# The weights' buffer of an expert's slot: chosen by a register in the products' addresses instead of by a branch between two copies of the code

## What is computed

```python
def _moe2_ref(x, w_gate, w_output_gate, w1, w2):
    logits = x @ w_gate                    # x: 2304 x 512
    e_idx = np.argmax(logits, axis=1)      # one of 8 experts for each token
    ...
    for e in range(E):
        mask = e_idx == e
        h = np.maximum(x[mask] @ w1[e], 0.0)   # 512 -> 1024
        ye = h @ w2[e]                         # 1024 -> 512
        out[mask] = gate_w[mask, None] * eom[mask, e, None] * ye
```

## Time and profile before

| what | us |
|---|---|
| median of three runs | 857.03 |
| the profiled execution, its own time | 863.49 |
| its span, first to last instruction | 861.7 |
| PE busy | 827.6 (96%) |
| VectorE busy | 572.5 (66%) |
| ScalarE busy | 383.6 (45%) |
| GpSimd busy | 180.2 (21%) |
| slots 3 to 26, first product to the last row of products | 636.3 to 851.3 |

### The profile page before, as it was taken

How to read it: one execution, slowest core, us unless ns; L and a number is a source line. 1 busy time by engine, 2 the same in 40 slices (tenths; PEclk the granted TensorE clock), 3 DMA queues, 4 the chain that set the end, 5 groups by cost and what they waited for, 6 DMA issues and landing times.

```text
span 861.7 us, 19310 instructions
## 1 busy us (share of the span) xinstructions
PE 827.6 (96%) x7018; PEld 549.2 (64%) x7019; DVE 572.5 (66%) x1200; ACT 383.6 (45%) x798; POOL 180.2 (21%) x208
## 2 busy tenths in 40 slices
PE   7999999999999999999999999999899999999995
PEld 5888777876555555555455555556577767777773
DVE  4778788877887998998898898855532444222221
ACT  5766667776555555555555555523111111111110
POOL 4444376663000001001001001010121222111100
PEclk9999999999999999999999999999999999999998
DMA  7255565541483884875784875485253852656610
GB/s 223 98 178 180 166 205 181 177 136 61 172 286 132 267 257 173 267 258 172 256 256 183 256 256 183 162 300 193 92 182 139 313 197 76 238 201 219 233 70 14
DMA packets 76554, 163.83 MB, mean 190 GB/s; under 512 B 39574, under 2 KB 43926, under 8 KB 69840
## 3 DMA queue, kind: packets, MB, share of 16 engines
q1 hardware_dynamic: 70576, 146.20, 50.3%
q0 software_dynamic: 5760, 16.80, 5.7%
q10 hardware_dynamic: 160, 0.07, 0.0%
HBM read 109.44 MB, written 47.47 MB: 182 GB/s over the span
## 4 chain that ended last, share of the span: by engine, by line
PE 70%; DVE 12%; issue 6%; DMA 5%; ACT 3%; POOL 2%; another core or an unknown queue 1%; DVEq 0%; POOLq 0%; ACTq 0%; SPq 0%
PE ps L876 18%; PE ps L865 15%; PE ps L971 11%; PE ps L959 11%; DMA arena<-split 4%; PE ps L781 4%; PE ps L726 3%; PE ps L753 3%; ACT arena L1073 2%; DVE arena L1256 2%; DVE arena L1510 2%; POOL arena L555 1%; PE ps L740 1%; DVE yrow L1475 1%; DVE relu L1566 1%
## 5 line engine op out<-in xcount | busy, mean ns | idle before, releaser
L865 PE MATMUL ps<-arena,w_in_sb 128*128 128x384 f16 x1152 | 200.9, 326 | 0.0
L876 PE MATMUL ps<-w_out_sb,arena 128*128 128x512 f16 x576 | 171.2, 379 | 5.0 <-DVE stage L1571 4.9
L865 PEld LDWEIGHTS ps<-arena,w_in_sb 128*128 128x128 f16 x1152 | 112.3, 98 | 80.9
L959 PE MATMUL ps<-x_sb,arena 128*128 128x128 f16 x2112 | 121.7, 219 | 3.9 <-DMA arena<-split 3.0
L959 PEld LDWEIGHTS ps<-x_sb,arena 128*128 128x128 f16 x2112 | 119.3, 98 | 8.1 <-issue 4.9
L1233 ACT ACTIVATE x_sb<-ps 128x512 f16<-128x512 f32 x54 | 31.6, 596 | 206.7 <-PE ps L959 172.4
L971 PE MATMUL ps<-arena,x_sb 128*128 128x512 f16 x528 | 119.7, 383 | 2.2 <-DVE x_sb L1667 2.2
L876 PE MATMUL ps<-w_out_sb,stage 128*128 128x512 f16 x288 | 109.1, 379 | 0.0
L1073 ACT ACTIVATE arena<-ps,arena 128x128 f32<-128x128 f32 x288 | 79.4, 382 | 55.4 <-DVE arena L1258 51.2
L1205 ACT ACTIVATE arena<-relu 128x384 f16<-128x384 f32 x96 | 50.0, 521 | 109.5 <-DVE relu L1566 108.3
L876 PEld LDWEIGHTS ps<-w_out_sb,arena 128*128 128x128 f16 x576 | 55.8, 98 | 65.4 <-issue 7.2
(11 more groups left out here) (210 smaller groups left out, 976.9 us busy)
## 6 DMA issues: line engine op xcount, KB each, us to landing
arena<-split SPq DMA_DIRECT2D x36, 1024.0 KB
arena<-in_moe_w SPq DMA_DIRECT2D x16, 2048.0 KB
split<-arena SPq DMA_DIRECT2D x16, 2048.0 KB, 7.5
arena<-in_qkt SPq DMA_DIRECT2D x15, 576.0 KB, 6.2
stage<-in_moe_w_in SPq DMA_DIRECT2D x16, 512.0 KB, 4.1
stage<-in_moe_w_out SPq DMA_DIRECT2D x16, 512.0 KB, 5.3
x_sb<-rows POOLq DMA_DIRECT2D x27, 257.0 KB
arena<-in_v SPq DMA_DIRECT2D x32, 128.0 KB, 4.4
```

The source lines that it names most:

```text
L865: last = nc.tensor.matmul(ps[:, HB[f % GB], 0:BN], w_in_sb[:, lw, c, f * P:(f + 1) * P], xt[:, a, lx, c, :], start=c == 0 and lw + lx == 0 ...
L876: last = nc.tensor.matmul(ps[:, YB + r, :], g_sb[lg_][:, f % GB, r * P:(r + 1) * P], w_out_sb[:, lw, f, :], start=f == 0 and lg_ + lw == 0 ...
L959: last = nc.tensor.matmul(ps[:, bank, f % 4 * P:(f % 4 + 1) * P], w1_sb[b][:, lw, c, f * P:(f + 1) * P], xgt[:, a, lx, c, :], start=c == 0 ...
```

## The change

Both copies of a used slot become one. The buffer `b` is no number of the code any more but the register `parity`, and the address of each piece of weights is worked out from it on the chip. The early slots still pass a number, and keep their fixed addresses.

```diff
+            def w1_of(b, lw, c, f):
+                if isinstance(b, int):
+                    return w1_sb[b][:, lw, c, f * P:(f + 1) * P]
+                return whole[:, bass.ds(b * (4 * UW) + ((lw * DC + c) * EF + f * P), P)]
+
+            def w2_of(b, lw, f):
+                if isinstance(b, int):
+                    return w2_sb[b][:, lw, f, :]
+                return whole[:, bass.ds(b * (4 * UW) + (2 * UW + (lw * EFC + f) * DM), DM)]
...
-                                                    w1_sb[b][:, lw, c, f * P:(f + 1) * P], xgt[:, a, lx, c, :],
+                                                    w1_of(b, lw, c, f), xgt[:, a, lx, c, :],
...
-                        last = nc.tensor.matmul(ps[:, 6 + a, :], hg[:, a, lh, f, :], w2_sb[b][:, lw, f, :],
+                        last = nc.tensor.matmul(ps[:, 6 + a, :], hg[:, a, lh, f, :], w2_of(b, lw, f),
...
-                    with pe.If(parity):
-                        used_slot(s, a, turn, more, need, 1)
-                    with pe.Else():
-                        used_slot(s, a, turn, more, need, 0)
+                    used_slot(s, a, turn, more, need, parity)
```

## The result

The change made the kernel slower. The median of four runs is 898.75 us (898.57 to 899.37) against 858.53 us for the kernel before beside it: a ratio of 1.0464, with a 95% interval of 1.0425 to 1.0503. That is 40.2 us more; 914 were forecast, with 873 to 973 as range. The profiled execution of after took 898.68 us, and its span is 896.9 us. In the lines of after L969 is L959 of before, L981 is L971, L978 is L968 and L1038 is L1028.

What follows compares the result with a forecast made beforehand. The array bounds the kernel before; the sequencer would bound the changed stage, with a period of 13.8 us, 15.9 with an empty slot. The stage's 57.4 us over the 857.0 median gave 914.4, rounded to 914; range 873 to 973.

Steps and rivals of the forecast that it cites:

- The bound: In the experts' stage the array sets the pace now; after the change PE's sequencer would, 0.281 us against 0.168 per three products.
- The groups: 80 added groups of register operations a slot, 64 in first products and 16 in second, each costing PE's sequencer 0.10 us.
- Loads and products: In the first products, each register-addressed weight load costs the sequencer 0.022 us and each product 0.005 us.
- The rest of the period: Sequencer work per slot beside 9.0 us of first products, giving a period of 13.8 us, 15.9 with an empty slot.
- The half of the second products: Half of a slot's second products costs the sequencer 4 x 0.281 = 1.12 us before the next slot.
- the way into the next slot: From leaving the block to the next slot's products: 1.8 us in the mean, 3.9 with an empty slot between.
- The sum of 57.4: Stage loss in us: 2.8 for the first used slot, then 3.7, 19.5 and 31.4 for two, five and eleven intervals.
- lower case: Engine instructions with register addresses cost the sequencer 0.005 us: period 12.0 us, loss 23 us, time 880 us.
- A: Not slower: a group costs only its record, about 0.05 us, three products 0.13, hidden under the array; 855 to 857; chance 0.08.
- B: Much slower: a register-addressed load costs PE's sequencer 0.05 to 0.10 us, giving 973 to 1076 us; chance 0.10 above 0.05.
- C: A gain: without the second copy, jumps over it are short; at most 1.6 us saved, 855 us; chance 0.02.
- What would show it: Signs in PE's profile: rows of 96 about 9 us, gaps put down to the sequencer, period 13 to 15 us, second products unchanged.

Runs made afterwards that it cites:

- two addresses: The change with only two register addresses, 2 groups in place of 64, for a slot's 96 first products: 857.84 us, ratio 1.0009 to the kernel before.
- The runs with smaller copies: Two runs against the kernel before: only second products by register, 864.53 us (1.0083); only their second half, the branch choosing copies of the rest, 863.26 us (1.0027).
- the first products alone: The change with only first products by register, second products in two copies behind a branch: 892.07 us, ratio 1.0403; with fixed-address second products and no branch, 893.55 us.
- the last run: Against the kernel before, only the second half of the second products by register, the branch choosing copies of the rest: 863.26 us, ratio 1.0027.

## Why the prediction was right, and where its terms were off

**The bound.** Right: the array set the pace before, and the sequencer does now. 64 groups take 8.2 us against 5.4 us of the array, and with the groups taken away (two addresses) the time is that of before.

**The groups.** The term was 0.100 us each, after four register instructions in a row. It is 0.124, and 0.128 with every eighth: a record of 0.046 and 0.078 beside it where engine instructions stand between two groups, against some 0.05 to 0.06 between register instructions alone. By this term the forecast was too low, 64 x 0.028 = 1.8 us a slot.

**Loads and products.** The terms were 0.022 for a load with an address from a register, after VectorE, and 0.005 for a product, after 24 instructions in 0.1 us: 0.081 for three. They are nothing that can be measured: groups with two and with four engine instructions between them keep the same pitch, and 96 register-addressed loads without groups run at the array's pace. By this step the forecast was too high, 32 x 0.081 = 2.6 us a slot. This is the step that failed: the room of half of 0.2 us was read as a price for each instruction, and VectorE's remainder as a price for its address. On PE no such price shows beside a pitch that is paid once for each register instruction; what VectorE's remainder is stays open. And the 0.2 us was no price in the first place: in finer digits the branch of L1031 starts at 738.327, 0.02 us after the array starts the seventh second product, and until then 35 instructions are handed on and not started, in 17 of the 19 slots alike. That is the limit that the experiments found, already at work in the kernel before. The two errors together leave 0.281 for three products against 0.256, 9.0 us for 96 against 8.2; that they nearly cancel is luck.

**The rest of the period.** The half of the second products was 1.12 and is 1.02 (8 groups, 779.96 to 780.98); the wait for the hidden values 1.5, and the second wait's record starts 1.6 us behind the end of the first products' groups; the way into the next slot 1.8, and is 2.0 and 1.6 in turn. With the measured 8.2 and 1.02 put in, the same sum is 8.2 + 1.5 + 0.1 + 1.02 + 1.8 + 0.1 + 0.15 = 12.87 us, against 12.83 in the trace. The forecast had 13.8, and 15.9 for 14.68 with an empty slot. The sum of 57.4 becomes 38.9: the eleven intervals 21.3 for 31.4, the five 12.9 for 19.5, the two 2.6 for 3.7, the single slot 2.2 for 2.8. Its lower case, 880 with engine instructions at 0.005, came with the group at 0.100 and is about as far off on the other side (19 us below, 914 is 15 above).

**The rivals.** A (not slower) fails because a group costs more than its record. Its deciding point, 0.202 us for three products, holds as far as it was tried: at 0.192 plain slots are at 11.05 us, and most of the loss lies where empty slots stand, as A's sum had it (5 us; 6.4 measured in all). B (a dear load) falls with the run of two addresses. The 62 ns that the Trainium skill has for a matmul whose decode is in microcode (page "TensorE: Matmul & The Clock Gate", section "Wait — 56ns, not 53.3ns?") would have given 997 by the prediction's estimate; no run here shows them, and with two addresses 96 register-addressed products start 0.056 us apart. C (a gain from the jumps) is right about its 1.6 us and finds no net time: in the run with two addresses the second products' groups lose as much behind empty slots, and in the change the first products' groups cost far more. The runs with smaller copies show that what a jump costs depends on how much work the array has queued ahead of it; moving it to a worse place was more than half of a loss of 7 us.

**What would show it.** Rows of about 9 us were expected, with gaps put down to the sequencer. The rows are 7.1 to 8.3 us, and there are no gaps: overlapping records hide them, so the place to look is the length of a row and the pitch of the groups. The period of 12.83 us lies just under the 13 to 15 that were named. The second products stayed at 5.3, the clock at 1.00, and the stage begins no later than it did (632.6 us, 636.3 before).

**What the sum left out.** A limit on how far the sequencer may run ahead. In the change it does not bind: the sequencer is 1.0 to 1.4 us ahead at the start of a slot, up to 11 groups, at the edge of the 35 instructions. With a shorter path it would have, and so the same sum fails for the first products alone: 21 us by it, 35 measured.

## What to carry to other kernels

Where an address comes from a register, count the register instructions that the build puts between the engine's instructions (the order shows them), and compare their pitch with the engine time between them: here 0.128 us against 0.084 us of array for each address, while the same groups between products of 0.22 us cost a plain slot nothing. A branch that is taken once for a whole block is cheap as long as the engine has enough work queued to cover its jump, so put it behind long instructions, and keep small, dense ones at fixed addresses. And do not trust an engine's busy share when its records overlap: compare how long the same row of instructions takes.

## What the runs showed of the hardware that was not expected

A group of register operations on PE costs its record and 0.078 us, as long as engine instructions stand between (0.046 to 0.124, 0.092 to 0.170, 0.153 to 0.232), and it makes no difference whether these are 2 or 4, or have an address from a register. Even the 16 of eight transposes fit in: L945's group starts at 778.249 with a record of 0.042, and the next register instruction at 778.369. Every eighth group or so is 0.03 us later.

The sequencer of PE hands on up to 35 engine instructions that the array has not started, and then waits. So a lead is worth 17 products, which is 1 us of first products and 3.7 us of second ones.

The first jump past another copy of the code held the sequencer for 3.0 us in the kernel before, 3.75 us in the last run, and 4.7 us where it stalled three instructions behind the jump. The Trainium skill says ("Runtime: NRT & Kernel Launch", section "Instruction fetch mechanics") that a taken branch to code outside the fetched window waits for its transfer. The trace agrees: each of the three stalls holds one packet of 16 KB in the DMA queue for instructions. The rows of the DMA view over the three stalls, in the same order (queue, packets, MB, share of 16 engines):

```profile
q8 instruction: 1, 0.02, 1.9%
...
q8 instruction: 1, 0.02, 1.5%
...
q8 instruction: 1, 0.02, 1.2%
```

In finer digits the sequencer goes on 1.4 us after the end of the packet in all three: 645.01 to 646.45, 644.35 to 645.79, 641.38 to 642.77. The 0.82 us of idle time at 652.02 in the kernel before also ends 1.3 us after such a packet (650.68). From 658.5 to 829 us that kernel has no such packet, and there no branch of L1029 takes more than 0.23 us. What the packets hold, and what the 1.4 us go to, no row shows.
